# A linear-attention, Fourier and two-MLP kernel: Fourier work moved one block later and spread over six blocks, zero matmuls moved and partly removed

## The reference, cut to what matters

```python
def _attn_ref(q, k, v, a_re, a_im):            # B, H, S, D = 4, 8, 768, 48
    ...                                        # a = (a_re, a_im), magnitude capped at 0.999
    for t in range(S):
        new_re = ar * S_re - ai * S_im
        new_im = ar * S_im + ai * S_re
        kv = np.einsum('bhd,bhe->bhde', k[:, :, t], v[:, :, t])
        S_re, S_im = (new_re + kv, new_im)
        y[:, :, t] = np.einsum('bhd,bhde->bhe', q[:, :, t], S_re)
    return y

def _moe_ref(x, w_ch1, w_ch2):                 # x: 4 x 768 x 384
    mixed = np.real(np.fft.fft(np.fft.fft(x, axis=1), axis=2))
    u = x + mixed
    un = (u - mean(u)) / np.sqrt(var(u) + 1e-06)
    return u + np.maximum(un @ w_ch1, 0.0) @ w_ch2      # 384 -> 1536 -> 384

def _moe2_ref(x, w_tok1, w_tok2, w_ch1, w_ch2):
    h = np.maximum(x.transpose(0, 2, 1) @ w_tok1, 0.0) @ w_tok2
    u = x + h.transpose(0, 2, 1)
    return u + np.maximum(u @ w_ch1, 0.0) @ w_ch2

# reference: _attn_ref, then _moe_ref, then _moe2_ref
```

## Time and profile before

| | us |
|---|---|
| median of three runs | 1056.67 |
| lowest, highest | 1048.11, 1070.27 |
| profiled execution | 1050.42 |
| its span | 1048.4 |
| TensorE matmul busy | 982.1 |
| VectorE busy | 514.9 |
| ScalarE busy | 357.8 |

### The profile page before, as it was taken

How to read it: one execution, slowest core, us unless ns; L and a number is a source line. 1 busy time by engine, 2 the same in 40 slices (tenths; PEclk the granted TensorE clock), 3 DMA queues, 4 the chain that set the end, 5 groups by cost and what they waited for, 6 DMA issues and landing times.

```text
span 1048.4 us, 15600 instructions
## 1 busy us (share of the span) xinstructions
PE 982.1 (94%) x6154; PEld 951.2 (91%) x6154; DVE 514.9 (49%) x940; ACT 357.8 (34%) x532; POOL 16.4 (2%) x12
## 2 busy tenths in 40 slices
PE   0389999999999999999999999999999999999997
PEld 0268889889899899999999999999999999999997
DVE  5888699999855654234324222542223214223220
ACT  7676666676531520220221221431213102121120
POOL 0000000000000000000000000030000000000000
PEclk9789899998999999999999999999999999999999
DMA  6689977986776064021021010010001001000000
GB/s 208 197 232 263 254 220 190 235 244 154 191 206 239 16 243 171 16 75 45 24 66 45 30 61 23 16 54 16 8 23 45 23 15 53 23 0 23 9 16 26
DMA packets 96745, 104.75 MB, mean 100 GB/s; under 512 B 13104, under 2 KB 90288, under 8 KB 96688
## 3 DMA queue, kind: packets, MB, share of 16 engines
q1 hardware_dynamic: 96688, 104.00, 33.6%
HBM read 70.86 MB, written 33.11 MB: 99 GB/s over the span
## 4 chain that ended last, share of the span: by engine, by line
PE 81%; DVE 8%; ACT 7%; issue 2%; DMA 0%; SPq 0%; DVEq 0%; ACTq 0%
PE bank L233 21%; PE bank L235 21%; PE bank L234 21%; PE bank L1173 3%; PE bank L1191 2%; DVE n_area L942 2%; PE bank L1189 2%; PE bank L1234 2%; PE bank L1250 2%; PE bank L1252 2%; PE bank L1202 2%; PE bank L1258 2%; PE bank L243 1%; DVE n_area L947 1%; DVE n_area L930 1%
## 5 line engine op out<-in xcount | busy, mean ns | idle before, releaser
L121 ACT ACTIVATE hh<-bank 128x384 fp32r<-128x384 f32 x192 | 94.5, 492 | 375.0 <-PE bank L235 375.0
L209 DVE SCALAR_TENSOR_TENSOR hl<-bank,hh 128x384 fp32r<-128x384 f32 x192 | 107.0, 557 | 195.6 <-ACT hh L121 195.6
L233 PE MATMUL bank<-w2h,hh 128*128 128x384 f32 x576 | 193.3, 336 | 0.0
L233 PE MATMUL bank<-nTh,w1h 128*128 128x384 f32 x576 | 193.0, 335 | 0.0
L235 PE MATMUL bank<-w2h,hl 128*128 128x384 f32 x576 | 192.5, 334 | 0.0
L234 PE MATMUL bank<-w2l,hh 128*128 128x384 f32 x576 | 192.5, 334 | 0.0
L235 PE MATMUL bank<-nTh,w1l 128*128 128x384 f32 x576 | 192.5, 334 | 0.0
L234 PE MATMUL bank<-nTl,w1h 128*128 128x384 f32 x576 | 192.4, 334 | 0.0
L233 PEld LDWEIGHTS bank<-nTh,w1h 128*128 128x128 f32 x576 | 108.1, 188 | 0.4 <-issue 0.2
L234 PEld LDWEIGHTS bank<-w2l,hh 128*128 128x128 f32 x576 | 108.2, 188 | 0.0
L234 PEld LDWEIGHTS bank<-nTl,w1h 128*128 128x128 f32 x576 | 108.1, 188 | 0.0
(11 more groups left out here) (156 smaller groups left out, 1294.1 us busy)
## 6 DMA issues: line engine op xcount, KB each, us to landing
w_area<-k_turn SPq DMA_DIRECT2D x24, 384.0 KB, 4.8
w_area<-q_turn SPq DMA_DIRECT2D x24, 384.0 KB, 6.1
q_turn<-w_raw SPq DMA_DIRECT2D x30, 192.0 KB, 3.0
k_turn<-n_area SPq DMA_DIRECT2D x24, 192.0 KB, 2.6
k_turn<-w_flat SPq DMA_DIRECT2D x24, 192.0 KB, 2.7
u_scratch<-h_area SPq DMA_DIRECT2D x24, 192.0 KB, 6.4
w_raw<-in_moe_w_ch SPq DMA_DIRECT2D x2, 2304.0 KB, 12.4
x_flat<-u_scratch SPq DMA_DIRECT2D x4, 1152.0 KB, 10.0
```

What stands on the lines that cost most here:

```text
L121: self.nc.scalar.activation(self.hh[:, m, :], self.mm_bank[(g * (KF + TPG) + m) % 2][:, 0:TG], ACT.Relu).then_inc(self.h_high, 1)
L209: self.nc.vector.scalar_tensor_tensor(out=self.hl[:, m, :], in0=self.mm_bank[(g * (KF + TPG) + m) % 2][:, 0:TG], scalar=0.0, in1=self.hh[: ...
L233: self.nc.tensor.matmul(out, lh, rh, start=(n == 0), stop=False)
```

## The change

The functions transformed_at and added_at now say: middle and widths in block j = 2, tiles 0 and 1 in j = 3, tile 2 in j = 4, tile 3 in j = 5, and tiles 4 and 5 in blocks j = 0 and j = 1 of the batch after. VectorE's fold stays in j = 1. Adds stand one block behind, as before. For batch 2, whose following batch has no blocks left after batch 3, tiles 3 to 5 end behind the loop: tile 3 is transformed in block 23 and added behind it, tiles 4 and 5 are transformed behind turn_y(23), into the state bank and the output bank, and added behind the last fold. The zero matmuls now stand behind turn_y, five in each of blocks 0 to 7, and none after. The one-element count takes another bank, and the wait for the wide tables moves from block 6 to 8.

```diff
--- before.py
+++ after.py
@@ -469,16 +469,18 @@
             if m:
                 turn_use["y", m - 1] = len(turn_use)
 
+        free_bank = tr_bank[1 - turn_use["y", NM - 1] % 2]
+
         def update_no(m):
             return (NCH - 1) * (m // NCH) + m % NCH
 
-        def transformed_at(j):
-            return {2: [0], 3: [1, 2], 4: [3, 4], 5: [5]}.get(j, [])
+        def transformed_at(m):
+            b, j = divmod(m, NCH)
+            n = b - 2 if j < 2 else b - 1
+            return [(n, i) for i in {3: [0, 1], 4: [2], 5: [3], 0: [4], 1: [5]}.get(j, []) if n >= 0]
 
         def added_at(m):
-            b, j = divmod(m, NCH)
-            n = b - 2 if j == 0 else b - 1
-            return [(n, i) for i in {3: [0], 4: [1, 2], 5: [3, 4], 0: [5]}.get(j, []) if n >= 0]
+            return transformed_at(m - 1) if m else []
 
         def products_done(p, i):
             return vec0[p.n] + 10 + 3 * p.chunks + 2 * (i // 2)
@@ -628,7 +630,8 @@
                     sp.dma_start(w2_early, slices(ap["moe_w_ch2"])).then_inc(w2_in, 16)
             for n, i in added_at(NM - 1):
                 store_u(n, i)
-            store_u(B - 2, 5)
+            for i in range(3, NT):
+                store_u(B - 2, i)
             for i in range(NT):
                 store_u(B - 1, i)
             for stored in out_stored:
@@ -816,7 +819,7 @@
                     evacuate_y(m - 1)
                 if (m, 2) in stage_at:
                     angle_tables()
-                if b and j == 1:
+                if b and j == 2:
                     middle(b - 1)
                     for n in range(KD):
                         widths(b - 1, n)
@@ -1002,11 +1005,12 @@
                     V.tensor_tensor(fold[:, 0, k_, 1:half], fwd, back, ALU.add)
                     V.tensor_tensor(fold[:, 1, k_, 1:half], fwd, back, ALU.subtract).then_inc(folded, 1)
 
-            def add_transform(b, i):
+            def add_transform(b, i, bank=None):
                 n = b * NT + i
+                bank = bank or f_bank[i % 2]
                 x = y_sb[:, n % YR, :]
                 dve.wait_ge(b_made, n + 1)
-                cc, sn = f_bank[i % 2][:, 0:FH], f_bank[i % 2][:, FH:2 * FH]
+                cc, sn = bank[:, 0:FH], bank[:, FH:2 * FH]
                 low, high = x[:, 0:FH], x[:, DM - 1:FH - 1:-1]
                 V.tensor_tensor(low, low, cc, ALU.add)
                 V.tensor_tensor(high, high, cc[:, 1:FH - 1], ALU.add).then_inc(b_half, 1)
@@ -1072,13 +1076,15 @@
                     ends(stage_at[m, 2])
                     tangents(stage_at[m, 2])
                     scaled(stage_at[m, 2])
-            add_transform(B - 2, 5)
+            add_transform(B - 2, 3)
             V.tensor_reduce(least[:, :], dstage[:, :, :, :], mybir.AxisListType.XYZ, ALU.min).then_inc(least_found, 1)
             dve.wait_ge(least_found, 1)
             V.tensor_scalar(at_floor[:, :], least[:, :], END_FLOOR, None, ALU.is_le).then_inc(floor_marked, 1)
             fold_sequence(B - 1)
+            add_transform(B - 2, 4, st_bank)
+            add_transform(B - 2, 5, y_bank)
             dve.wait_ge(floor_counted, 1)
-            V.tensor_copy(steep[:, :], st_bank[0:1, 0:1]).then_inc(steep_set, 1)
+            V.tensor_copy(steep[:, :], free_bank[0:1, 0:1]).then_inc(steep_set, 1)
             s0.low_normed(dve, 0, 0)
             s0.low_normed(dve, 0, 1)
             s0.low_w1(dve, 0)
@@ -1213,7 +1219,9 @@
 
             def middle(b):
                 pe.wait_ge(tr_free, turn_use["y", b * NCH + NCH - 1] + 1)
-                if b:
+                if b == B - 1:
+                    pe.wait_ge(b_added, (b - 1) * NT + 3)
+                elif b:
                     pe.wait_ge(b_added, b * NT - 1)
                 for k_ in range(KD):
                     last = mm(f_bank[0][0:1, 0:FH], yT[:, k_, S // 2:S // 2 + 1], cd[:, k_, :],
@@ -1223,7 +1231,9 @@
             def width_transform(b, m):
                 if m == 0:
                     pe.wait_ge(folded, (b + 1) * KD)
-                    if b:
+                    if b == B - 1:
+                        pe.wait_ge(b_added, (b - 1) * NT + 4)
+                    elif b:
                         pe.wait_ge(b_added, b * NT)
                 if m == 1:
                     pe.wait_ge(mid_ready, b + 1)
@@ -1236,15 +1246,16 @@
                                   start=(k_ == 0), stop=(k_ == KD - 1))
                 last.then_inc(a_made, 1)
 
-            def sequence_transform(b, m):
-                if m < 2:
-                    pe.wait_ge(a_ready, b * KD + 2 + m)
-                else:
-                    pe.wait_ge(b_added, b * NT + m - 1)
+            def sequence_transform(b, m, out=None):
+                if out is None:
+                    if m < 2:
+                        pe.wait_ge(a_ready, b * KD + 2 + m)
+                    else:
+                        pe.wait_ge(b_added, b * NT + m - 1)
+                    out = f_bank[m % 2]
                 if m == 0:
                     pe.wait_ge(a_ready, (b + 1) * KD)
                 rows = slice(m * P, (m + 1) * P)
-                out = f_bank[m % 2]
                 mm(out[:, 0:FH], alt, a_mid[:, :], start=True, stop=False)
                 for k_ in range(KD):
                     mm(out[:, 0:FH], cs[:, k_, rows], a_sb[:, k_, 0:FH], start=False, stop=(k_ == KD - 1))
@@ -1280,32 +1291,30 @@
                 pe.wait_ge(v_in[p.s], 16 * (p.turn + 1))
                 if j < NCH - 1:
                     update(m)
-                if m < NCH:
-                    keep_busy(5)
-                if m == NCH:
+                if m == NCH + 2:
                     pe.wait_ge(wide_tables_in, 5 * 16)
-                if b and j == 1:
+                if b and j == 2:
                     middle(b - 1)
                     for n in range(KD):
                         width_transform(b - 1, n)
-                if b:
-                    for n in transformed_at(j):
-                        sequence_transform(b - 1, n)
+                for n, i in transformed_at(m):
+                    sequence_transform(n, i)
                 if m:
                     turn_y(m - 1)
-                if b and j == 0:
-                    if b > 1:
-                        pe.wait_ge(b_added, (b - 1) * NT - 1)
-                    keep_busy(8)
+                if m < NCH + 2:
+                    keep_busy(5)
             wait_for_outputs(NM - 1)
             for h in range(H):
                 output(NM - 1, h)
             s0.transposes(pe, 0, 0)
             s0.transposes(pe, 0, 1)
             turn_y(NM - 1)
+            pe.wait_ge(st_free, B * (NCH - 1))
+            sequence_transform(B - 2, 4, st_bank)
+            sequence_transform(B - 2, 5, y_bank)
             pe.wait_ge(floor_marked, 1)
-            pe.wait_ge(st_free, B * (NCH - 1))
-            mm(st_bank[0:1, 0:1], at_floor[:, :], ones[:, :], start=True, stop=True).then_inc(floor_counted, 1)
+            pe.wait_ge(tr_free, turn_use["y", NM - 1])
+            mm(free_bank[0:1, 0:1], at_floor[:, :], ones[:, :], start=True, stop=True).then_inc(floor_counted, 1)
             middle(B - 1)
             width_transform(B - 1, 0)
             s0.transposes(pe, 0, 2)
```

## The result

The changed kernel took 1062.83 us in the median of 20 runs (1059.58 to 1072.52), the kernel before 1058.20 us in 20 runs (1048.11 to 1070.27). The ratio is 1.0093, with a 95% interval of 1.0067 to 1.0118: slower by a little, and inside 2%. That ratio leaves out runs more than 1.5% above the fastest of their kernel, which here takes away the slowest runs of the kernel before; over all of the 20 and 20 runs the means are 1065.0 and 1058.5 us, 6.5 us apart (3.3 to 9.7). In this document I compare means over all runs, because the clock is what they differ by. The forecast was 1057 us, range 1046 to 1072.

A forecast was written before the change was run, and what follows sets the result against it. VectorE and a ring VectorE, TensorE, ScalarE were taken to bound batches 1 and 2. Terms of 0, -0.1, +2.9, 0, +0.5 and 0 gave +3.3 us: 1053.7 by profile, 1060.0 by median, so 1057 us, range 1046 to 1072.

The forecast's parts named there:

- The bound of batches 1 and 2: Batches 1 and 2: VectorE and a ring VectorE, TensorE, ScalarE bound them; VectorE could gain about 4 us a batch.
- rival C: Clock falls at heads of batches 2 and 3, 1.4 to 5 us each; two more: 1063 to 1070 us; chance 0.20.
- The link of the ring: Batch 2: turn_y of block 14 releases the phases of block 15; widths between update and turn_y add 5.0 us.
- Batch 1, +2.9 us: Blocks 6 to 11: block 7's zeros follow a late turn_y; masking of 9 ends +4.1 us, less 1.2 for adds.
- Batch 2, -0.1 us: Blocks 12 to 17: masking of 15 ends 1.1 us later, fewer adds give back 1.2.
- Batch 0, 0 between -6 and +6.6: Turn_y ahead of the zeros: -6 us at best from VectorE's waits, +6.6 at worst in blocks 1 and 4; taken as 0.
- Batch 3 and the end, +0.5 us: From block 19's update on: -1.65 us with one tile fewer, +2.1 for tiles 4 and 5 behind the loop.
- The clock: The granted clock fell twice to half before; a fall was put at 1.4 to 5 us, with no term in the sum.
- B: Rival: TensorE bounds the kernel after all, so 9.3 us of net zeros come off: 1047 us, 1041 by the profile; chance 0.15.
- D: Rival: batch 0 gains both waits for ScalarE and all else stays, -6 us, 1054 us; chance 0.05.

The follow-up runs named there:

- the zeros in the stream: One zero matmul amid each block's narrow matmuls, added to the change with turn_y and arctangents earlier, zeros ahead of turn_y; mean 1061.7 us, 1.3 us faster.
- the version of the lowest mean: The change with turn_y ahead of the widths, arctangents ahead of two width copies, four zeros at the heads of batches 2 and 3; mean 1054.5 us.
- the Fourier move alone: The change's new places for tiles, middle and widths, with the zero matmuls where the kernel before had them; mean 1068.6 us, ratio 1.012.

## Why the prediction was right, and what in it was not

**The bound of batches 1 and 2: right in kind, not whole.** VectorE's wait for the arctangents grew from 1.2 to 7.3 and 10.9 us in blocks 9 and 15, where 4 or more was said. The wait of TensorE at turn_y of block 7 for the evacuation is there. That TensorE's added work is free beside VectorE is not so: the zeros in the stream cost 9 to 12 of their 14 us once the clock is set aside. Three other signs failed. VectorE's waits for TensorE's outputs (L1191, now L1197) in blocks 8 and 14 were to be gone and are 3.2 and 2.1 us. TensorE was to wait some 3 us for the masking at blocks 13 and 19, and its longest wait of that kind in the blocks is 1.0 us. And the clock was at half in five stretches, where more than two were to mean rival C.

**The link of the ring: wrong.** That turn_y of block 14 releases the phases of block 15 held in the kernel before, where the tile's copy was the last thing ahead of the arctangents. In the change the three width copies stand ahead of them in ScalarE's order, and moving turn_y alone left 7.2 us of wait. The count came out right (+5 us for the widths) since widths and turn_y end together.

**Batch 1, +2.9 us.** The profile has +5.1, with two falls in its window (143 to 150 and 201 to 215 us). Maskings 6 to 9 took 44.3 us instead of the 42.1 worked out, with the first fall in them; maskings 9 to 12 took 1.2 us less than before, as worked out. That block 7's zeros cost 3.3 us where they follow a late evacuation is borne out by the run with the zeros ahead of turn_y, 3.2 us less. What the term left out is the clock: taking the zeros of blocks 6 and 7 away costs 7.9 us.

**Batch 2, -0.1 us.** The profile has +8.3, with the fall of 228 to 246 us and most of that of 286 to 301. Maskings 12 to 15 took 50.0 us where 39.1 was worked out, with 16 us at half clock in them. The price at full clock was not seen in the change; the version of the lowest mean, with another order and eight zeros more, takes 74.0 us, about batch 1's 74.2 of the earlier trace rows.

**Batch 0, 0 between -6 and +6.6.** Blocks up to 6 end 2.4 us earlier than before, with 8 us at half clock instead of 11, which is worth up to 1.5 of them. Zeros ahead of turn_y give 139.4 instead of 134.8 us, of which up to 3 us are the clock's. So there was a gain of 1 to 2 us from the earlier turn_y, inside the bounds.

**Batch 3 and the end, +0.5 us.** The profile has +2.9 from block 18's masking on. The tiles behind the loop were done as described:

```profile
360.63 0.49 PE L1259 MATMUL bank<-late_area,tok_raw 128*128 128x193 f32 x2
362.92 0.49 PE L1259 MATMUL bank<-late_area,tok_raw 128*128 128x193 f32 x2
...
366.43 2.23 PE L1244 MATMUL bank<-res_area,w_area 128*128 128x193 f32 x12
```

From turn_y (360.25) to the first width it is 6.2 us, where it was 4.1: +2.1, as worked out. From the update of block 19 (305.25) to the start of the last tile ahead of the loop's end (353.38) it is 48.1 us, where it was 50.4: -2.3, where -1.65 was taken. Of the other 3.1 us, 2.5 lie at the head of batch 3: the update of block 19 starts 6.3 us after the masking of block 18 where it was 3.8, in the fall of 286 to 301 us.

**The clock: the step that was mis-sized.** The sum had nothing for it, and rival C, chance 0.20, had two more falls and +3 to 10. Over all runs the change has 15 us more at half clock (80 against 64), and with 0.50 us for each, from the runs of the kernel before, that is 7.7 us (6.3 with the 0.41 of the change's own runs): all of the 5.8 to 6.5 us by which the means differ. At equal time at half clock the two kernels are equal within 2 us by this estimate, where +3.3 was forecast. So the forecast came near the measured +4.6 of the medians partly by luck: terms that were too high at equal clock stood in for the clock's share, which had none.

Rival C was right in kind and not in mechanism. It wanted two more falls, in the narrow matmuls behind the place where the head zeros had stood. The change's profile has five instead of the two of the earlier trace rows. Two begin in blocks 12 and 18, but some 14 us ahead of that place (turn_y of these blocks is at 215.18 and 300.07 us), the others in blocks 1, 7 and 14. And with all head zeros back the Fourier move alone has 82 us at half clock. Why the move brings falls stays open. That over 2% takes five falls more was not put to the test, but even 107 us more at half clock, without any zeros, came to 1.4%.

The Trainium skill (TensorE: Matmul & The Clock Gate, Part 1, "What's actually happening") has a throttled default that activity releases. The run without zeros agrees, with 113 us at 0.50. What its rule leaves open is that TensorE's matmul records are busy for 110 of those 113 us.

**B and D.** B (TensorE bounds, -9.3) did not come about by the time, though the zeros in the stream indicate that its premise was not empty: TensorE's time is not free, and both engines bound these batches. D's gain in batch 0 was real in part: VectorE's waits for the arctangents there went from 2.9 and 3.0 us to none and 1.1, but it now waits 4.2 us for TensorE in block 2, where the zeros follow a late evacuation.

## What to carry to other kernels

When work moves from one block to another, follow it through the order of every engine that copies its result: here the three copies on ScalarE, not the matmuls, held back the gate work of the next block, and putting the urgent instructions ahead of two of them took 4 us off the wait. Filler matmuls are a cost and a hold on the clock at once, so weigh their removal by the time at half clock over many runs, not by one profile. And where a kernel's runs spread by 2%, plot time against mean granted clock first: in the kernel before, one slope accounted for the spread.

## What the runs showed of the hardware that was not expected

The granted clock can fall with almost no idle time ahead of it (6.75 of 7.00 us busy in 245 to 252 us of the kernel before, longest wait 0.25 us), and it can stay low with TensorE's records busy for 110 of 113 us, without zeros. Taking away the two idle times of 3.8 us at turn_y did not take away the falls; one 384-column matmul amid the narrow ones of each block took the time at half clock from 80 to 54 us. A us at half clock goes with 0.50 us of the kernel's time on 93 runs of the kernel before (0.24 to 0.62 in the others, with 6 to 20 runs each). The same program had between 42 and 88 us at half clock from run to run; how much it gets is not fixed by the program alone.
